# A gap of 448 bytes ahead of the second weight buffer of a two-network feed-forward kernel

## What is computed

```python
def _attn_ref(q, k, v, g_norm):
    kv = np.einsum('bhsd,bhse->bhde', k, v)
    out = np.einsum('bhsd,bhde->bhse', q, kv)
    rms = np.sqrt(np.mean(out * out, axis=-1, keepdims=True) + 1e-06)
    return out / rms * g_norm

def _moe_ref(x, w_in, w_out):
    h = x @ w_in
    return (h * (1.0 / (1.0 + np.exp(-1.702 * h)))) @ w_out

def _moe2_ref(x, w_in, w_out):
    h = x @ w_in
    return (np.maximum(h, 0.0) + np.log1p(np.exp(-np.abs(h)))) @ w_out
```

## Time and profile before

| | before |
|---|---|
| median of 3 runs | 882.18 us |
| lowest, highest | 882.14, 883.94 us |
| span of the profiled execution | 881.6 us |
| TensorE, matmuls | 861.9 us busy, 98% |
| VectorE | 438.1 us busy, 50% |
| ScalarE | 268.0 us busy, 30% |
| GpSimd | 205.4 us busy, 23% |
| mean granted TensorE clock | 0.991 |

### The profile page before, as it was taken

How to read it: one execution, slowest core, us unless ns; L and a number is a source line. 1 busy time by engine, 2 the same in 40 slices (tenths; PEclk the granted TensorE clock), 3 DMA queues, 4 the chain that set the end, 5 groups by cost and what they waited for, 6 DMA issues and landing times.

```text
span 881.6 us, 11362 instructions
## 1 busy us (share of the span) xinstructions
PE 861.9 (98%) x4064; PEld 714.6 (81%) x4064; DVE 438.1 (50%) x769; ACT 268.0 (30%) x493; POOL 205.4 (23%) x173
## 2 busy tenths in 40 slices
PE   6999999999999999999997999999999999999997
PEld 5877888888888888888995888888888888888896
DVE  1487443433343334333587644564456445644564
ACT  3555320211021102110344433343334333433343
POOL 1459530000000000000297322132213221322132
PEclk9999999999999999999997999999999999999999
DMA  8935420000000000000052000100010001000100
GB/s 295 301 144 170 141 72 0 1 1 1 1 0 0 0 0 0 0 0 0 25 186 102 1 1 1 48 0 0 0 48 0 0 0 48 0 0 0 48 2 24
DMA packets 13868, 36.55 MB, mean 41 GB/s; under 512 B 1552, under 2 KB 3600, under 8 KB 13840
## 3 DMA queue, kind: packets, MB, share of 16 engines
q1 hardware_dynamic: 13840, 36.18, 12.0%
HBM read 31.46 MB, written 4.72 MB: 41 GB/s over the span
## 4 chain that ended last, share of the span: by engine, by line
PE 95%; DVE 2%; issue 1%; DMA 1%; ACT 1%; POOLq 0%; POOL 0%; ACTq 0%; DVEq 0%; SPq 0%
PE ps L379 44%; PE ps L407 44%; PE ps L306 3%; PE ps L317 2%; PE ps L331 1%; DMA tail_sb<-k_v 1%; DVE xs L603 1%; PE ps L343 0%; DVE gs L657 0%; DVE xy L589 0%; DVE hid L575 0%; DVE xs L605 0%; ACT sq_sb L468 0%; DVE inv_s L577 0%; DVE gs L659 0%
## 5 line engine op out<-in xcount | busy, mean ns | idle before, releaser
L657 DVE CAST gs<-hid 128x512 fp32r<-128x512 f32 (+1 forms) x160 | 76.1, 476 | 292.4 <-PE ps L407 291.0
L379 PE MATMUL ps<-xs,w_own 128*128 128x512 f32 (+1 forms) x960 | 211.2, 374 | 4.5 <-DVE xs L605 4.3
L379 PE MATMUL ps<-xs,w_shared 128*128 128x512 f32 (+1 forms) x960 | 214.7, 372 | 0.0
L379 PEld LDWEIGHTS ps<-xs,w_own 128*128 128x128 f32 x960 | 170.5, 192 | 37.8 <-DVE xs L605 6.5
L379 PEld LDWEIGHTS ps<-xs,w_shared 128*128 128x128 f32 x960 | 168.5, 188 | 35.0
L283 POOL TENSOR_TENSOR stage<-stage 128x512 f32<-128x512 f32 (+1 forms) x80 | 94.6, 1183 | 298.1 <-DVE stage L641 298.1
L513 ACT ACTIVATE hid<-ps 128x512 f32<-128x512 f32 (+1 forms) x80 | 44.5, 557 | 272.8 <-PE ps L379 250.2
L659 DVE TENSOR_TENSOR gs<-hid,gs 128x512 fp32r<-128x512 f32 (+1 forms) x160 | 115.8, 724 | 5.5
L266 POOL TENSOR_TENSOR w_own<-stage,w_own 128x512 fp32r<-128x512 f32 x32 | 42.6, 1366 | 314.8 <-ACT w_own L456 314.8
L517 ACT ACTIVATE stage<-ps 128x512 f32<-128x512 f32 (+1 forms) x80 | 44.5, 557 | 206.9 <-PE ps L379 193.0
L407 PE MATMUL ps<-gs,w_shared 128*128 128x512 f32 (+1 forms) x480 | 105.5, 373 | 0.8 <-DVE gs L657 0.6
(11 more groups left out here) (42 smaller groups left out, 443.3 us busy)
## 6 DMA issues: line engine op xcount, KB each, us to landing
stage<-moe_w SPq DMA_DIRECT2D x32, 512.0 KB, 3.3
kv_in_sb<-k_v SPq DMA_DIRECT2D x16, 512.0 KB, 5.5
q_sb<-q_t SPq DMA_DIRECT2D x16, 288.0 KB, 4.6
out<-xy SPq DMA_DIRECT2D x18, 256.0 KB, 2.2
tail_sb<-k_v SPq DMA_DIRECT2D x4, 256.0 KB, 6.0
xy<-head_bcast SPq DMA_DIRECT2D x1, 512.0 KB, 7.3
g_col<-g_norm SPq DMA_DIRECT2D x2, 0.2 KB, 6.0
```

Of the source, the lines that this page charges most:

```text
L379: mm = nc.tensor.matmul(bank, w[:, W_IN, wp, cols], xs[:, xp, k, 0:width], start=(k == 0 and (wp, xp) == (HI, HI)), stop=(k == KT - 1 and ...
L657: nc.vector.tensor_copy(gs[:, HI, s, :width], g).then_inc(g_hi_made, 1)
```

## The change

A tile that nobody writes or reads is allocated behind `eps_col`, ahead of the attention's tiles and of `w_shared`. It is 448 bytes in each partition, so the attention's tiles and `w_shared` lie 448 bytes higher. No instruction is added or removed.

```diff
         gs = sb("gs", [P, 2, HID_SLOTS, CHUNK], F32R)
         g_col = sb("g_col", [P, 1], F32)
         eps_col = sb("eps_col", [P, 1], F32)
+
+        sb("phase_gap", [P, (512 - 64) // 4], F32)
 
 
         with ExitStack() as att:
```

## The result

| | before | after |
|---|---|---|
| median | 882.59 us (4 runs) | 869.86 us (4 runs) |
| lowest, highest | 882.14, 883.94 us | 868.05, 871.28 us |
| ratio, 95% interval | | 0.9853 (0.9838 to 0.9868) |
| span of the profiled execution | 881.6 us | 868.2 us |
| mean granted TensorE clock in it | 0.991 | 0.997 |

The changed kernel is 1.5% faster. Three later groups of runs of the same two kernels gave ratios of 0.9878 (0.9864 to 0.9893), 0.9870 (0.9853 to 0.9887) and 0.9861 (0.9840 to 0.9881), with medians of the changed kernel of 871.11, 870.30 and 869.95 us. So the gain is some 11 to 13 us where the sum had 9.1.

What follows compares the result with a forecast made beforehand. TensorE's feed-forward matmuls were taken as the bound, busy 98% of the span. Savings of 5.56 and 4.36 us less losses of 0.44 and 0.35 gave 9.13 us less: forecast 873.0 us, range 870.6 to 876.0.

Steps and rivals of the forecast that it cites:

- the sum: Total of the forecast's gains and losses over the whole kernel: 5.56 + 4.36 - 0.44 - 0.35 = 9.13 us less.
- Items 1 and 2: Full 512-token chunks, first and second feed-forward networks: every 12-matmul piece at 2.72 us, saving 5.56 and 4.36 us.
- Items 3 and 4: 256-token remainders of the first and second networks: pieces on `w_shared` take `w_own`'s longer times, losing 0.44 and 0.35 us.
- Item 5: Attention part: all its tiles move together, so operand distances stay; zero taken, with 1.6 us either way possible.
- Item 6: GpSimd's subtraction making the weights' low parts, 1366 ns into `w_own`, 1412 into `w_shared`: perhaps 46 ns gained, zero taken.
- Item 7: Turn from first to second network, where TensorE waits for `xs` and its clock halves: zero taken, bounds 1.6 us either way.
- the place: Rival: `w_shared` is slow because it lies high in memory, so the gap changes nothing; 882.2 us, chance 0.07.
- the dear equal phase: Rival: place explains the 2.80 us pieces and equal operand addresses modulo 512 cost extra; 886.8 us, chance 0.04.
- the half effect: Rival: `w_shared` settles at another cadence than `w_own`, or only the first network gains; 877.4 us, chance 0.07.
- rule of two independent read ports: Rival: loading weights takes no read bandwidth from the running matmul, so addresses can't meet and nothing changes; a small chance.

## Why the prediction was right, and where it was wrong

- *Items 1 and 2, the full chunks*: right in mechanism and size, 5.53 and 4.36 us less for 5.56 and 4.36. The first chunk was priced like the others, rightly.
- *Items 3 and 4, the remainders*: right. Every piece took the longer value of `w_own`; the last stretch is 0.31 us longer for 0.35.
- *Item 5, the attention*: right at zero (ratio 1.0003 with only its tiles moved).
- *Item 6, GpSimd's low parts*: 1396 ns into the moved buffer for 1412 in the earlier trace rows. `w_own`, which did not move, changed by as much (1379 for 1366), so no part of the 46 ns is shown to be the address. Zero was right here in size.
- *Item 7, the turn*: this step failed, "I take zero". With the remainder's 0.44 the sum had the stretch 0.44 us longer; it was 1.93 shorter, 2.37 off. I had seen half a clock and waits for `xs` there, and bounded only the clock, at 1.6 us either way. That price was right (1.65 us when the clock alone differed). But I took the casts of `xs` for granted, although five of VectorE's eight rows of that stretch were far too long in the trace of before: three casts of 1.5 us for 0.42, two subtractions of 1.64 for 0.69. The last split came 1.83 us earlier against the remainder's first `down` (477.82 + 1.64 - 429.51 = 49.95 before, 468.58 + 1.63 - 422.09 = 48.12 after, by the matmuls' starts), although the remainder itself was slower: from its first `down` to TensorE's first stop it took 36.01 us for 35.67. A slower step was added in full, as 0.44 us, to a stretch that ends on another chain. The traces show what moved the casts: one `gs` cast began 0.35 us later and met GpSimd (1.43 us for 0.47), and the two together put the casts of `xs` 1.3 us later, into GpSimd's pause. It met GpSimd by 0.02 us only, if in all eight profiles alike, and no row that I had read of before told that it would. The pace of the remainder brings this and takes it away (1.41 us pieces lost it at the same address), while 0.47 us more work at the old pace did not bring it.
- *The sum*: with 1.93 less in the place of 0.44 more it is 11.5 us, 870.7 from the first median. That lies just inside my range. The last 0.7 us to the 12.2 that the four groups gave on average (12.7, 11.2, 11.7, 13.4) is within what the clock's falls, at the start and at the turn, put on or take off single executions; that is argued, not shown. The measured 869.86 fell below the low end, 870.6, because the sum had no term for a gain at the turn beyond the clock; how far below it fell is in part luck.
- *The rivals*: the place, the dear equal phase and the half effect all fell, by the gap of 512 bytes and by the periods. The Trainium skill's rule of two independent read ports (page "TensorE: Matmul & The Clock Gate", section "Step-by-step: what each phase is for") doesn't hold in the sense in which I had weighed it: the address of the one operand against the other changes the cadence by 6.6 ns a matmul (2.80 for 2.72 us), with nothing else changed. What in the chip makes the two addresses meet, no run shows.

## What to carry to other kernels

When TensorE is the bound and the profile shows the same matmul at two cadences, compare the addresses of the stationary and the moving operand: here the equal address modulo 256 bytes was the best at 512 columns, one gap tile took 9 us of 882 off the matmuls (and 2 more off the turn), which two small tiles of 32 bytes ahead of a large buffer had cost. Test it with the buffer moved by a whole period, which must change nothing. And where a stretch ends on a chain of other engines, a change of TensorE's pace moves how they meet: read the durations of single casts there (0.42 or 1.5 us) before taking the stretch as fixed.

## What the runs showed of the hardware that I had not expected

- The cadence of fp32r matmuls of 512 columns depends on the distance of the two operands' addresses with a period of 256 bytes: 226.7 ns a matmul at equal address, 229 at 64 below (233 there in some chunks, beside slower neighbours), 232.1 to 234.2 elsewhere; never 213 ns, which is half of the 427 at half clock. It holds whichever of the two buffers is the stationary one.
- At 256 columns equal address is not the best (120 ns a matmul in the first remainder, 113.3 at 192, 320 and 448 bytes), and one distance (448) ran at 113.3 in one kernel and 117.8 in another.
- A VectorE cast of 0.42 us beside GpSimd's two-input subtractions takes 1.5, a two-input operation of 0.69 takes 1.64. One such meeting, of 1 us, made the turn shorter, because it moved the casts that followed into GpSimd's pause.
- The granted clock fell at the turn in some executions of the same program and not in others, worth 1.65 us, and for 3.4 us near 63 us, where the first `down` came at 80.5 to 81.5 us with the fall and at 79.0 to 79.7 without.
